# Packed attention and two feed-forward layers on one core: a new order from attention to the first two blocks, own tiles for the last batch, high parts first in the last block, and tiles at equal alignment

## The reference

```python
scale = 1.0 / np.sqrt(64)
def sm_attn(qq, kk, vv):                  # softmax attention
    s = scale * np.matmul(qq, kk.transpose(0, 1, 3, 2))
    a = np.exp(s - np.max(s, axis=-1, keepdims=True))
    a = a / (np.sum(a, axis=-1, keepdims=True) + 1e-09)
    return np.matmul(a, vv)
# q, k, v: (8 batches, 8 heads, 576, 64); p: (8, 8, 32, 64)
p_packed = sm_attn(p, k, v)               # 32 packed queries per head
x = sm_attn(q, p_packed, p_packed)        # every query attends to the 32 packed rows
x = x.transpose(0, 2, 1, 3).reshape(4608, 512)
h = x @ w_in                              # 512 -> 1024
e = np.exp(h - h.max(-1, keepdims=True))
solu = h * (e / (e.sum(-1, keepdims=True) + 1e-09))
ln = (solu - mean) / np.sqrt(var + 1e-06) * g_ln
x = ln @ w_out                            # 1024 -> 512
h = np.maximum(np.maximum(x @ w1, x @ w2), x @ w3)   # 512 -> 768
out = h @ w_out2                          # 768 -> 512
```

## The kernel before

| matmuls | stationary operand | moving operand |
|---|---|---|
| `up` | `a_even`, `a_odd`: 0 | `m_even`, `m_odd`: 0 |
| `down` | `w_out_s`: 96 | `ln`: 96 |
| `up3` with w1 | 64 | `ys`: 96 |
| `up3` with w2, w3 | 0 | `ys`: 96 |
| `down2` | `h2`: 96 | `w_out2_s`: 96 |

## Time and profile before

### The profile page before, as it was taken

How to read it: one execution, slowest core, us unless ns; L and a number is a source line. 1 busy time by engine, 2 the same in 40 slices (tenths; PEclk the granted TensorE clock), 3 DMA queues, 4 the chain that set the end, 5 groups by cost and what they waited for, 6 DMA issues and landing times.

```text
span 1157.3 us, 14217 instructions
## 1 busy us (share of the span) xinstructions
PE 1121.8 (97%) x5938; PEld 896.5 (77%) x5938; DVE 466.2 (40%) x798; ACT 338.6 (29%) x555; POOL 145.0 (13%) x133
## 2 busy tenths in 40 slices
PE   7999998799999999998999999999999999999998
PEld 5776675588888888886888888887888888788887
DVE  3675777566576566553221222222122222212121
ACT  5556664243244144222111121212112121211211
POOL 0011353311233020218000000000000000000000
PEclk9899999899999999999999999999999999999999
DMA  9977852301331221103202020010202011010000
GB/s 259 319 223 216 251 189 104 133 37 75 112 112 37 75 107 41 55 15 113 73 1 73 1 73 1 28 46 1 73 1 73 1 37 37 8 66 1 37 0 37
DMA packets 65198, 90.83 MB, mean 78 GB/s; under 512 B 19696, under 2 KB 44272, under 8 KB 63472
## 3 DMA queue, kind: packets, MB, share of 16 engines
q1 hardware_dynamic: 61648, 73.81, 20.3%
q0 software_dynamic: 3488, 16.13, 3.9%
HBM read 61.21 MB, written 30.80 MB: 80 GB/s over the span
## 4 chain that ended last, share of the span: by engine, by line
PE 91%; DVE 3%; ACT 3%; DMA 1%; issue 1%; POOL 0%; SPq 0%; ACTq 0%
PE ps L996 39%; PE ps L569 26%; PE ps L1004 12%; PE ps L744 2%; PE ps L921 2%; PE ps L578 2%; PE ps L714 2%; PE ps L789 1%; DMA k_raw<-in_k_dram 1%; PE ps L673 1%; ACT ost L1265 1%; DVE ln_lo L1300 1%; ACT a2T L1037 1%; ACT packed L1113 1%; PE ps L768 0%
## 5 line engine op out<-in xcount | busy, mean ns | idle before, releaser
L996 PE MATMUL ps<-ys_lo,w_s_hi 128*128 128x512 f32 x648 | 256.7, 396 | 0.7 <-ACT yst L1037 0.7
L996 PE MATMUL ps<-ys_hi,w_s_lo 128*128 128x512 f32 x648 | 256.7, 396 | 0.0
L996 PE MATMUL ps<-ys_hi,w_s_hi 128*128 128x512 f32 x648 | 255.4, 394 | 0.0
L1534 DVE TENSOR_TENSOR second<-ps,first 128x512 f32<-128x512 f32 x54 | 37.3, 692 | 319.5 <-PE ps L996 319.5
L996 PEld LDWEIGHTS ps<-ys_hi,w_s_lo 128*128 128x128 f32 x648 | 121.8, 188 | 29.9
L996 PEld LDWEIGHTS ps<-ys_lo,w_s_hi 128*128 128x128 f32 x648 | 121.8, 188 | 29.8 <-ACT yst L1037 1.1
L996 PEld LDWEIGHTS ps<-ys_hi,w_s_hi 128*128 128x128 f32 x648 | 121.7, 188 | 29.8
L1037 ACT ACTIVATE h_hi<-third 128x512 fp32r<-128x512 f32 x54 | 34.1, 632 | 313.1 <-DVE third L1538 313.1
L569 PE MATMUL ps<-ln_lo,w_out_s_hi 128*128 128x512 f32 x288 | 112.8, 392 | 3.1 <-DVE ln_lo L1300 3.1
L569 PE MATMUL ps<-ln_hi,w_out_s_lo 128*128 128x512 f32 x288 | 113.2, 393 | 0.0
L569 PE MATMUL ps<-ln_hi,w_out_s_hi 128*128 128x512 f32 x288 | 113.1, 393 | 0.0
(11 more groups left out here) (130 smaller groups left out, 1411.0 us busy)
## 6 DMA issues: line engine op xcount, KB each, us to landing
y_features<-yst SPq DMA_DIRECT2D x9, 1024.0 KB, 4.5
y_raw<-y_features SPq DMA_DIRECT2D x9, 1024.0 KB, 5.3
out_dram<-ost SPq DMA_DIRECT2D x36, 256.0 KB, 2.1
k_raw<-in_k_dram SPq DMA_DIRECT2D x32, 256.0 KB, 6.1
v_raw<-in_v_dram SPq DMA_DIRECT2D x8, 1024.0 KB, 6.4
q_raw<-in_q_dram SPq DMA_DIRECT2D x32, 256.0 KB, 5.3
m_merged<-merged POOLq DMA_DIRECT2D x6, 1024.0 KB, 5.1
weight_raw<-in_moe_w_dram POOLq DMA_DIRECT2D x9, 512.0 KB, 4.4
```

Source lines behind the costliest of these rows:

```text
L996: last = pe.matmul(ps[:, 3 * (c % 2) + w, :], w_max3[w][a][:, kk, c * P:(c + 1) * P], ys[z][:, kk, :], start=(kk == 0 and e == 0), stop=(k ...
L1534: dve.tensor_tensor(tmp2[c % 2][:, :], ps[:, 3 * (c % 2) + 1, :], tmp1[c % 2][:, :], ALU.max)\
```

## The change

- `place` puts every tile of 2048 bytes or more at a multiple of 128 bytes, and the bases `w1_base` and `MIDDLE` move to such multiples. All operands of the table above then start at 0 modulo 128. Modulo 256 they are equal too; modulo 512 `w1_s` equals `ys`, while w2 and w3 differ from it by 256.
- The last batch gets tiles of its own, `merged_last` and `a2T_last`, in the places of `v_raw` and `a1T`, which nobody reads any more by then. Its copies no longer wait for stores.
- `scores2(b, 0)` waits for two parts of the batch before instead of three, `scores2(b, 1)` still for three. For batches 0 and 1 DVE makes `lo_a(b, 2)` before `lo_m(b, 0)` instead of after it.
- `last_step` has a new order on PE, ACT and DVE, `up(1, 1)` moves into it, and DVE makes `moments(0, 1)` to `moments(0, 3)` after all four `lo_t(0, i)`. `turn_h(0, 0)` goes to bank 0.
- `down(8, 0)` makes its 16 matmuls with `ln_hi` first, as soon as the four high parts are there, and the 8 with `ln_lo` after that. It writes bank 0.
- Stage 3 starts when `y_copied` has counted 33; the wait for all 36 moves to the first `down2`.

The diff, cut to its changed lines and their neighbours:

```diff
@@ -66,6 +66,8 @@
             size *= n
+        if size >= 2048:
+            cursor[0] = (cursor[0] + 127) // 128 * 128
         t = nc.alloc_sbuf_tensor_at(name, shape, dt, offset=cursor[0])
@@ -97,11 +99,12 @@
     late_scale = place("late_scale", [P, ALL_TILES])
-    w1_base = cursor[0]
+    w1_base = (cursor[0] + 127) // 128 * 128
+    cursor[0] = w1_base
     w1_s = place_split("w1_s", [P, KM, FF2])
-    MIDDLE = 98272
+    MIDDLE = 98176
     assert cursor[0] <= MIDDLE
@@ -120,8 +123,10 @@
     qT = place("qT", [P, PAIRS * S])
+    merged_last_base = cursor[0]
     v_raw = place("v_raw", [P, H, FULL, D])
     v_tail = place("v_tail", [P, H, D])
+    a2T_last_base = cursor[0]
     a1T = place("a1T", [P, TILES, QUADS, P])
@@ -152,6 +157,10 @@
     merged = place("merged", [P, QUADS, FF1])
+    cursor[0] = merged_last_base
+    merged_last = place("merged_last", [P, QUADS, FF1])
+    cursor[0] = a2T_last_base
+    a2T_last = place("a2T_last", [P, QUADS, S])
@@ -330,7 +339,16 @@
     def t_bank(t, i):
-        return (2, 0, 4, 6)[i] if t == 0 else 2 * i
+        return 2 * i
+    def y_bank(t, m):
+        return 0 if t == BLOCKS - 1 and m == 0 else 6 + m % 2
+    def merged_of(b):
+        return merged_last if b == B - 1 else merged
+    def a2T_of(b):
+        return a2T_last if b == B - 1 else a2T
@@ -498,12 +516,12 @@
                 wait_alone(pool, a2T_copied, S2_PARTS * b + S2_PARTS)
-                pool.dma_start(a_dram[b], a2T[:, :, :]).then_inc(a_stored, 16)
+                pool.dma_start(a_dram[b], a2T_of(b)[:, :, :]).then_inc(a_stored, 16)
...
                 wait_alone(pool, m_copied, QUADS * b + QUADS)
-                pool.dma_start(m_dram[b], merged[:, :, :]).then_inc(m_stored, 16)
+                pool.dma_start(m_dram[b], merged_of(b)[:, :, :]).then_inc(m_stored, 16)
@@ -733,9 +751,9 @@
-                    pe.wait_ge(a2T_copied, S2_PARTS * b)
+                    pe.wait_ge(a2T_copied, S2_PARTS * (b - 1) + 2 + n)
                     if b <= 2:
-                        pe.wait_ge(a_low, S2_PARTS * b)
+                        pe.wait_ge(a_low, S2_PARTS * (b - 1) + 2 + n)
                 if n == 2:
@@ -825,7 +843,7 @@
-                    pe.wait_ge(t_split, TPB * (t - 1) + (i + 1 if t > 1 else 2))
+                    pe.wait_ge(t_split, TPB * (t - 1) + i + 1)
                 else:
@@ -910,6 +928,9 @@
+                    pe.wait_ge(h_used, 2)
+                elif t == 0 and i == 1:
                     pe.wait_ge(a2T_copied, S2_PARTS * B)
@@ -924,11 +945,26 @@
+                if t == BLOCKS - 1 and m == 0:
+                    pe.wait_ge(t_split, TPB * t + 1)
+                    pe.wait_ge(t_hi, TPB * t + TPB)
+                    for w in w_out_s:
+                        for c in range(K1):
+                            pe.matmul(ps[:, y_bank(t, m), :], w[:, c, 0:P], ln[0][:, c, :], start=w is w_out_s[0] and c == 0,
+                                      stop=False)
+                    pe.wait_ge(t_split, TPB * t + TPB)
+                    for c in range(K1):
+                        last = pe.matmul(ps[:, y_bank(t, m), :], w_out_s[0][:, c, 0:P], ln[1][:, c, :], start=False,
+                                         stop=c == K1 - 1)
+                    last.then_inc(y_filled, 1)
+                    return
                 pe.wait_ge(t_split, TPB * t + TPB)
...
                     pe.wait_ge(y_copied, KM * t + m - 1)
-                three_passes([(ps[:, 6 + m % 2, :],
+                three_passes([(ps[:, y_bank(t, m), :],
                                [([w[:, c, m * P:(m + 1) * P] for w in w_out_s],
@@ -941,15 +977,16 @@
                 scores2(b, 2)
+                up(0, 2)
                 turn_a2(b, 1)
-                up(0, 2)
+                turn_h(0, 0)
+                up(0, 3)
                 turn_a2(b, 2)
-                up(0, 3)
-                turn_h(0, 0)
                 turn_h(0, 1)
...
                 turn_h(0, 3)
+                up(1, 1)
@@ -957,7 +994,7 @@
                     up(t, 0)
-                up(t, 1)
+                    up(t, 1)
                 down(t - 1, 0)
@@ -1008,10 +1045,16 @@
             def block3(t, first):
+                if first:
+                    pe.wait_ge(y_copied, KM * (BLOCKS - 1) + 1)
                 for c in range(K2):
...
                 pe.wait_ge(h2_split, K2 * t + K2 - 1)
+                if first:
+                    pe.wait_ge(y_copied, KM * BLOCKS)
                 wait(pe, o2_copied, TPB * t)
@@ -1025,7 +1068,6 @@
-            pe.wait_ge(y_copied, KM * BLOCKS)
             block3(0, True)
@@ -1085,18 +1127,18 @@
                 else:
-                    if n == 0 and b > 2:
+                    if n == 0 and 2 < b < B - 1:
                         act.wait_ge(a_stored, 16 * (b - 2))
-                    dst = a2T
+                    dst = a2T_of(b)
                 copy(a2T_cols(dst, n), a2T_src(n)).then_inc(a2T_copied, 1)
...
                 act.wait_ge(m_filled, QUADS * b + g + 1)
-                if g == 0 and b > 2:
+                if g == 0 and 2 < b < B - 1:
                     act.wait_ge(m_stored, 16 * (b - 2))
-                dst = m_s[b][:, 0, g, :] if b < 2 else merged[:, g, :]
+                dst = m_s[b][:, 0, g, :] if b < 2 else merged_of(b)[:, g, :]
                 bank = wide_banks[g]
@@ -1194,7 +1236,7 @@
                 act.wait_ge(y_filled, KM * t + m + 1)
-                copy(yst[:, m, :], ps[:, 6 + m % 2, :]).then_inc(y_copied, 1)
+                copy(yst[:, m, :], ps[:, y_bank(t, m), :]).then_inc(y_copied, 1)
@@ -1219,12 +1261,12 @@
                 exp_h(0, 1)
+                exp2(b, 2)
                 copy_a2(b, 1)
-                exp2(b, 2)
                 exp_h(0, 2)
+                hi_t(0, 0)
                 copy_a2(b, 2)
                 exp_h(0, 3)
-                hi_t(0, 0)
                 hi_t(0, 1)
@@ -1422,8 +1464,8 @@
                 if direct:
+                    lo_a(b, 2)
                     lo_m(b, 0)
-                    lo_a(b, 2)
                     lo_m(b, 1)
@@ -1505,13 +1547,16 @@
                 inverse2(b, 2)
-                moments(0, 1)
-                for i in range(2, TPB):
-                    max_h(0, i)
-                    solu(0, i)
+                max_h(0, 2)
+                solu(0, 2)
+                lo_t(0, 0)
+                max_h(0, 3)
+                solu(0, 3)
+                lo_t(0, 1)
+                lo_t(0, 2)
+                lo_t(0, 3)
+                for i in range(1, TPB):
                     moments(0, i)
-                for i in range(TPB):
-                    lo_t(0, i)
```

## The result

| | before | after |
|---|---|---|
| median, us | 1158.53 | 1120.21 |
| lowest and highest run | 1158.1, 1159.57 | 1119.91, 1121.4 |
| profiled execution, device time | 1159.12 | 1120.02 |
| its span | 1157.3 | 1118.2 |

The ratio is 0.9667, with a 95% interval of 0.9644 to 0.969. The forecast was 1123.8 us with a range of 1120.5 to 1136.5; the time lies 3.6 us under the forecast and 0.3 us under the range. The direction was right and the terms were there; the size of one, the alignment, was too small, and the rule behind it was not the right one. The medians differ by 38.3 us and the spans by 39.1, where the sum had 34.7.

The account below looks back on a forecast made before the run. PE, busy 97% of the span, was taken as the bound: idle or low-clock time and matmul distance. 13.9 - 0.3 + 3.0 + 1.6 + 1.9 + 1.8 + 0.6 + 12.2 = 34.7 us off 1158.51 gives 1123.8, range 1120.5 to 1136.5.

Parts of the forecast that it names:

- Equal alignment: In `up3`, operands starting at the same address modulo 128 bring matmuls from 233.5 to 227.2 ns: 12.2 us, bounds 0 to 14.
- The rule behind it: Matmuls are fast where both operands start at the same address modulo 128 bytes, slow in `up3` where they differ.
- Hand-over, 13.9: From attention to the blocks: own tiles and the new order start `down(0, 0)` earlier, 13.9 us gained.
- The wait at `turn_h(0, 1)`: Between attention and the blocks, PE waits 0.3 us for a copy queued on ACT.
- The late `lo_t(1, 0)`, -0.3: At the end of block 1's `up`, moments put last may make this low part late, 0.3 us lost.
- First batches, 3.0 + 1.6: At `scores2(1, 0)` and `scores2(2, 0)`: waits 1.5 us shorter each, 3.0; clock staying up after the second, 1.6.
- The bounds for the clock, 0 and 1.6: After the second early `scores2` wait, PE's clock staying at 2.4 GHz gains between 0 and 1.6 us.
- Last block, 1.9 + 1.8 + 0.6: Block 8: `ln_hi` matmuls start earlier, 1.9 us; clock stays up, 1.8; the `yst` wait ending stage 2 goes, 0.6.
- two rivals of the alignment: In `up3`: alignment does nothing, 1136.0 us, chance 0.20; only a third gained, by addresses modulo 512, 1131.9 us, chance 0.10.
- The case of the clock: Rival: both clock falls, in the first batches and last block, stay; 1127.2 us, chance 0.13.
- that of the order: Rival: ACT and DVE bind between attention and blocks, 5 us lost, last block's clock falls; 1130.6 us, chance 0.12.

Follow-up runs that it names:

- two pairs of kernels: Kernel before with only the rounded-up tile places and bases: 1144.17 us, against the kernel before; changed kernel without them: 1137.97 us, against the changed kernel.

## Why the prediction was right and wrong

The step that failed is the term "Equal alignment": its mechanism held, but it was put at 12.2 us and measured 14.7, more than the 14 that it had as an upper bound. With 14.7 the sum is 37.2 us and the time 1121.3, inside the range. The 1.1 us that are then left are about what the two profiled executions differ by in the first 50 us, 1.2, which the working took as fixed; whether the medians differ there too isn't shown.

- **Alignment, 12.2.** The mechanism was right and the term too small: 14.7 measured, by two pairs of kernels (14.6 by the second). Two things failed in its working. The price of a matmul was taken as 233.5 - 227.2 = 6.3 ns, with a floor that leaves slow matmuls at each change of kind in place; by the chain it is (50.44 - 48.96) / 216 = 6.85 ns, 13.3 us for 1944. And the 1.2 us of stage 2 stood only in the bound of 14, though most of them could be counted from the trace of before: nine matmuls at each of 23 changes, 41 to 48 ns each time. "The others keep what they have: their operands were equal and stay so" is the sentence that failed: each pair was equal, but the pairs were not equal to each other.
- **The rule behind it.** "Equal modulo 128" agreed with all rows of before and is not the rule; 256 is. The kernel met 256 as well, so the term didn't suffer. Rows 9 and 10 held two pairs at equal places (`up` and `down`) and the unlike ones of `up3`, too few to tell a period.
- **Hand-over, 13.9.** Right to 0.1 us: the working put `down(0, 0)` at 213.3 less 4.6, 208.7 us; it starts at 207.34, and the attention ahead of it is 1.5 shorter than forecast. The wait at `turn_h(0, 1)` was put at 0.3 and is 0.5. The moments run from 207.0 to 211.6.
- **The late `lo_t(1, 0)`, -0.3.** It didn't come; PE has no wait for `ln_lo` at all, and 132 matmuls from 204.78 to 234.71 run in one piece.
- **First batches, 3.0 + 1.6.** 4.9 measured from the first product on. The other 1.2 us of that stretch are not of the sum, and no step of the working allowed for the start: the trace of before was taken as the place from which to count, while executions of the same program differ by up to 2.7 us there. The bounds for the clock, 0 and 1.6, followed the one trace of before, where it falls once: of the four other kernels with the old waits one did the same, two fell twice and one never, so that the hit at 1.6 is in part luck.
- **Last block, 1.9 + 1.8 + 0.6.** 4.3 forecast, 4.3 measured. The Trainium skill ("TensorE: Matmul & The Clock Gate", Part 4: PE-mode transpose) would have had the 32 transposes count against the clock and the 1.8 be lost. The stretch of 500 to 512 us is at 1.00 after 3.5 us of transposes and 1.3 idle, so here the trace doesn't bear that out; the fall followed a longer idle time, 3.1 to 3.2 us, and not always.
- **The range.** The forecast's own low end, 1121, had 14 for the alignment and 14.4 for the hand-over, and the stated one, 1120.5, lies only 0.5 below it. The former was too low by 0.7 and nothing stood for the start. Its high end was held up by two rivals of the alignment, 0.30 together, that none of the runs supports. The case of the clock and that of the order didn't occur: no granted clock below 1.00 at the two places, and one wait of 0.5 us at the hand-over.

The errors all had one sign: 2.5 alignment, 1.2 start, 0.3 first batches, 0.3 for the wait that didn't come, 4.3 of the 4.4 us that the spans show beyond the sum.

## What to carry over

Where one matmul of a kind is slower than another of the same shape, compare the start addresses of weights and moving operand: in fp32r with 128x512 each, a difference that isn't a multiple of 256 bytes cost 2.5 to 3% here, and placing all large tiles at one phase also removed the slow matmuls at each change between `up` and `down`, though not those behind transposes. Count a rate's gain from the whole groups in the chain, down to the fastest one seen, and look for the same loss inside the groups that seem fast. Before comparing two traces, cut them at instructions that both have, since the first 50 us alone differ by more than some of the terms.

## What the hardware showed that was not expected

- The distance between 128x512 fp32r matmuls was 226.7 ns with both operands at the same address modulo 256, 232.4 with 128 bytes between them, and 233.3 with 32 or 64.
- After a change from a pair at one place to a pair at another, 96 bytes on, nine matmuls were slow by 41 to 48 ns in all, in the same pattern each time; 128 bytes on, one by 4 ns. Behind transposes slow matmuls came even with all large operands at one address modulo 256.
- The clock's fall after an idle time isn't certain: after the same wait it came in four of five kernels, at two places of the program alike, and at a third in two of five.
- The first 50 us differ by up to 3.7 us between traces, and the later starts go with 6.8 us at 1.2 GHz there instead of 3.4.
